# An attention and two gated feed-forward layers on one core: q's column norms taken over all partitions at once, before the softmax

## The chip, the cores and the metric

The kernel runs on one core of one Trainium2 chip. The metric is the device time of one execution in microseconds (us), smaller is better. Times of the kernel before are the median of three runs; the profile is of one more execution.

## The reference

Only the first stage matters here. q, k and v are 6016 x 256 in float32.

```
qn = q / (norm of each column of q + 1e-06)
kn = k / (norm of each column of k + 1e-06)
s  = kn.T @ qn / tau                  # 256 x 256
s  = s - s.max(-1);  a = exp(s);  a /= a.sum(-1) + 1e-09
x  = v @ a                            # 6016 x 256
x  = x / rms(x) * gain;  y = (silu(x @ w_gate) * (x @ w_val)) @ w_out      # layer 1, d_ff 1536
out = (sigmoid(y @ w2_gate) * (y @ w2_val)) @ w2_out                       # layer 2
```

## The kernel before, in words

Five instruction streams are written out by hand, each in its own order, and are tied by semaphores. TensorE (PE) does the products; float32 products run in two passes, and where it pays a matrix is split in a rounded high part and a low rest (float32r). VectorE (DVE) and ScalarE (ACT) do the elementwise work, GpSimd (POOL) a little, SyncE (SP) issues nearly all DMAs.

**The stream of q and k.** Twenty-four pieces of q and k come in. ACT squares them (L461), DVE adds the squares (L694, folded at L707), and PE adds each piece into the raw scores k.T @ q, which lie in two PSUM banks, RAW: 128 rows (c = 0) and 128 rows (c = 1) of 256 columns. The last four pieces (LATE) are done for c = 0 first; ahead of the last of them PE makes the column sums of the squares (`column_norms`, L1087): four small float32 products, each with 128 columns of squares as the held matrix and one column of ones moving, which leave 128x1 in each of four banks (L1093). When c = 0 is whole (`raw_done` 1), PE does c = 1 of the first late piece, waits for `soft_step` 2, spreads q's inverse norms over all partitions (`spread_columns`, L1078, two products with the identity), and does c = 1 of the three other pieces (`raw_done` 2).

**From the sums to the scale.** ACT takes the root of the 128x4 sums (L473); DVE refines it and inverts it: reciprocal (L808), product with the sums (L811), sum (L814), reciprocal (L817, `half_inv`), k's own scale (L820, `k_scale`). Each step waits for the one before it.

**The softmax, two row halves.** `score(0)` (L834) multiplies the spread norms in PSUM by an SBUF copy of the raw scores (made by ACT, L475), by k's scale, and keeps each row's maximum; L838 negates it. ACT takes the exponents (L526), DVE inverts the row sum (L844, L847), ACT writes the first half of a (L532). ACT also copies the spread norms to SBUF (L543) for `score(1)`, which reads the raw scores from PSUM. v's first block arrives in `v_in` and is turned by DVE in two halves, `turn_v(0, 0)` and `turn_v(0, 1)` (L667), each of which bumps `v_turned`; ACT rounds the second half (L443), DVE makes its low part (L685). PE's `first_x` (L1017) multiplies the first half of v by the first half of a in float32 (L1023), once `v_turned` is 1 and a's half is there, and then waits for the second half of a (L852, L857) for the products of L1028. The order on DVE is: k_scale, turn_v(0,0), score(0), turn_v(0,1), inverse_sum(0), score(1), vt_low(0,1), inverse_sum(1), second_a.

**Behind it.** `first_up` (L1042) is the first tile of layer 1; the row norms of block 0 come from `add_squares(0)` on DVE (L729) and `sum_squares` on PE (L1071). DVE's `turn_v(1, 0)` stands just ahead of `add_squares(0)`. On SP, `load_v(1)` (L317) waits for `v_turned` 2, and the remaining weight loads stand behind it. From there on the twelve blocks of 512 tokens go through both layers in an order that is the same before and after.

Of the kernel before, what the change touches and what calls it, by code (L numbers as in the profile page):

```python
# [26 lines left out]
ALU = mybir.AluOpType  # L27
ACT = mybir.ActivationFunctionType
AX_X = mybir.AxisListType.X

P = 128
# [10 lines left out]
LATE = (21, 22, 23, 20)  # L42
# [7 lines left out]
def build(nc, q, k, v, tau, rms_g, w1_gate, w1_val, w1_out, w2_gate, w2_val, w2_out, out):  # L50
    _, N, C = q.shape
    F = w1_gate.shape[1]
    CC = C // P
# [42 lines left out]
    def alternate(cols, h):  # L96

        return cols[:, h:C:CC]
# [5 lines left out]
    with ExitStack() as ctx:  # L104
# [3 lines left out]
        def sem(name):  # L108
            return ctx.enter_context(nc.semaphore(name))
# [11 lines left out]
        with ExitStack() as early:  # L121
            qk = early.enter_context(nc.sbuf_tensor("qk", [P, QK_SLOTS, 2, QK_TILES * C], F32))
            sq_qk = early.enter_context(nc.sbuf_tensor("sq_qk", [P, SQ_BUFS, 2, QK_TILES * C], F32))
            sum_sq = early.enter_context(nc.sbuf_tensor("sum_sq", [P, 2, QK_TILES * C], F32))
# [6 lines left out]
        ones = sb("ones", [P, P])  # L131
# [7 lines left out]
        scratch = sb("scratch", [P, CC, BLOCK])  # L139
        y1 = sb("y1", [P, CC, BLOCK])  # L140
# [9 lines left out]
        small = sb("small", [P, 64])  # L150
# [3 lines left out]
        ps = ctx.enter_context(nc.psum_tensor("ps", [P, 8, BLOCK], F32))  # L154
        GATE, VALUE = (0, 2), (1, 3)
        Y, X = (4, 5), (6, 7)
        RAW, NORM, SPREAD = (0, 1), (2, 3, 4, 5), 2
        sum_ps = ps[:, X[0]:X[1] + 1, :]
        square_sums = ps[:, NORM[0]:NORM[3] + 1, 0:1]

        gain = [cols_t[:, c * SQ:c * SQ + 1] for c in range(CC)]
        tau_c = cols_t[:, 2 * SQ:2 * SQ + 1]
        qk_hi = [w_hi["o1"][:, n * JG:(n + 1) * JG, :].rearrange("p (a t) c -> p a (t c)", a=2) for n in range(HI_BUFS)]

        seed = small[:, 0:4]
        seed_inv = small[:, 4:8]
        other = small[:, 40:44]
        twice_norm_e = small[:, 44:48]
        four_inv_tau = small[:, 52:53]
        unread = small[:, 48:49]  # L170
        tiny = halves[:, 0, 0:1]
        half_inv = small[:, 12:16]
        inv_tau = small[:, 16:17]
        k_scale = small[:, 18:20]
        neg_max = small[:, 22:24]
# [4 lines left out]
        ms = small[:, 32:36]  # L180
        rinv = small[:, 36:40]

        q_scale = y1[:, 0, 0:C]
        first_raw = y1[:, 0, C:2 * C]
        scores = y1[:, 1, :].rearrange("p (c m) -> p c m", c=CC)
        probs = h[:, 0, :].rearrange("p (c m) -> p c m", c=CC)
        first_a = scores[:, 0, :]
        sq = scratch
        mean, root_y, root_t, root_turned = (roots[0:SQ, i, :] for i in range(4))
        ROOT_STEPS = 9 + 3 * ROOT_ROUNDS  # L190
        late_root = y1[:, 1, :]
# [14 lines left out]
        raw_done, sums_folded = sem("raw_done"), sem("sums_folded")  # L206
        norms_made, root_seeded, root_refined = sem("norms_made"), sem("root_seeded"), sem("root_refined")
        first_hi_done = {w: sem(f"first_hi_{w}") for w in W[:2]}
        first_lo_done = {w: sem(f"first_lo_{w}") for w in W[:2]}
        soft_step, q_spread, q_scaled = sem("soft_step"), sem("q_spread"), sem("q_scaled")  # L210
        raw_copied = sem("raw_copied")
        scores_neg_max, exp_done, row_inv_ready = sem("scores_neg_max"), sem("exp_done"), sem("row_inv_ready")
        first_a_done, a_hi_done, a_lo_done = sem("first_a_done"), sem("a_hi_done"), sem("a_lo_done")
        first_a_hi_done, first_a_lo_done = sem("first_a_hi_done"), sem("first_a_lo_done")
# [207 lines left out]
        def _(act):  # L422
# [47 lines left out]
              .then_inc(first_hi_done["g1"], 1)  # L470
            act.wait_ge(const_ready, 4)
            act.wait_ge(norms_made, 1)
            nc.scalar.activation(seed.unsqueeze(2), square_sums, ACT.Sqrt, bias=tiny).then_inc(root_seeded, 1)  # L473
            act.wait_ge(raw_done, 1)
            nc.scalar.activation(first_raw, ps[:, RAW[0], 0:C], ACT.Copy).then_inc(raw_copied, 1)  # L475
            act.wait_ge(table_loaded, 1)
            nc.scalar.activation(unread, ones[:, 0:1], ACT.Exp).then_inc(table_loaded, 1)

# [59 lines left out]
                  .then_inc(a_hi_done, 1)  # L538

            exponents(0)  # L540
            act.wait_ge(q_spread, 1)
            act.wait_ge(soft_step, 4)
            nc.scalar.activation(q_scale, ps[:, SPREAD, 0:C], ACT.Copy).then_inc(q_scaled, 1)  # L543
            first_a_scaled()
            vt_high(0, 1, x2)
            exponents(1)
# [102 lines left out]
        def _(dve):  # L649
# [13 lines left out]
            def turn_v(b, c):  # L663
                w = width(b)
                if c == 0:
                    dve.wait_ge(v_loaded, b * 16 * QUARTERS + 16 * QUARTERS)
                nc.vector.transpose(x_raw[:, c, 0:w].rearrange("p (s t) -> p s t", t=SQ),  # L667
                                    v_in[:, 0:w // SQ, c:C // QUARTERS:CC]).then_inc(v_turned, 1)
# [131 lines left out]
            def x2_low(b, c, dst):  # L800
# [7 lines left out]
            nc.vector.reciprocal(seed_inv, seed).then_inc(root_refined, 1)  # L808
            dve.wait_ge(root_refined, 1)
            dve.wait_ge(norms_made, 1)  # L810
            nc.vector.tensor_tensor(other.unsqueeze(2), square_sums, seed_inv.unsqueeze(2), ALU.mult)\  # L811
              .then_inc(root_refined, 1)
            dve.wait_ge(root_refined, 2)
            nc.vector.scalar_tensor_tensor(out=twice_norm_e, in0=other, scalar=2e-6, in1=seed, op0=ALU.add, op1=ALU.add)\  # L814
              .then_inc(soft_step, 1)
# [1 line left out]
            nc.vector.reciprocal(half_inv, twice_norm_e).then_inc(soft_step, 1)  # L817
            dve.wait_ge(soft_step, 2)
            dve.wait_ge(cols_made, 4)
            nc.vector.tensor_scalar(k_scale, half_inv[:, 2:4], four_inv_tau, None, ALU.mult).then_inc(soft_step, 1)  # L820
            turn_v(0, 0)
            dve.wait_ge(soft_step, 3)

            def score(c):

                if c:
                    dve.wait_ge(q_scaled, 1)
                    dve.wait_ge(raw_done, 2)
                    in_psum, in_sbuf = ps[:, RAW[1], 0:C], q_scale
                else:  # L830
                    dve.wait_ge(raw_copied, 1)
                    dve.wait_ge(q_spread, 1)
                    in_psum, in_sbuf = ps[:, SPREAD, 0:C], first_raw
                nc.vector.tensor_tensor_reduce(out=scores[:, c, :], in0=in_psum, in1=in_sbuf,  # L834
                                               scale=k_scale[:, c:c + 1], scalar=LOWEST, op0=ALU.mult, op1=ALU.max,
                                               accum_out=row_max[:, c:c + 1]).then_inc(soft_step, 1)
                dve.wait_ge(soft_step, 2 * c + 4)
                nc.vector.tensor_scalar(neg_max[:, c:c + 1], row_max[:, c:c + 1], -1.0, None, ALU.mult)\  # L838
                  .then_inc(scores_neg_max, 1)

            def inverse_sum(c):

                dve.wait_ge(exp_done, c + 1)
                nc.vector.tensor_scalar(row_sum_e[:, c:c + 1], row_sum[:, c:c + 1], 1e-9, None, ALU.add)\  # L844
                  .then_inc(soft_step, 1)
                dve.wait_ge(soft_step, 2 * c + 5)
                nc.vector.reciprocal(row_inv[:, c:c + 1], row_sum_e[:, c:c + 1]).then_inc(row_inv_ready, 1)  # L847
# [11 lines left out]
                                                   op0=ALU.mult, op1=ALU.subtract).then_inc(a_lo_done, 1)  # L859

            score(0)
            turn_v(0, 1)
            inverse_sum(0)
            score(1)
            vt_low(0, 1, x2)
            inverse_sum(1)
# [5 lines left out]
            for back in range(2):  # L872
                for d in range(CC):
# [3 lines left out]
                                                   in1=xs[0][:, d, tokens].bitcast(F32), op0=ALU.mult, op1=ALU.subtract)\  # L877
# [115 lines left out]
        def _(pe):  # L993
# [81 lines left out]
            def spread_columns(bank, cols, n):  # L1075

                for i in range(n):
                    mm = nc.tensor.matmul(ps[:, bank, i * P:(i + 1) * P], cols[:, i:i + 1].broadcast_to([P, P]),  # L1078
                                          ident[:, :], start=True, stop=True)
                return mm  # L1080
# [6 lines left out]
            def column_norms():  # L1087

                pe.wait_ge(sums_folded, 1)
                for part in range(2):  # L1090
                    cols = sum_sq[:, part, 0:C]
                    for c in range(CC):
                        mm = nc.tensor.matmul(ps[:, NORM[2 * part + c], 0:1],  # L1093
                                              alternate(cols, c) if part else cols[:, c * P:(c + 1) * P],
                                              ones[:, 0:1], start=True, stop=True)
                mm.then_inc(norms_made, 1)

            def warm_up(n):

# [4 lines left out]
            def raw(i, c, first=0, end=QK_TILES):  # L1104

                _, slot, t0, n = chunks[i]
                dst = ps[:, RAW[c], 0:C]
                for t in range(first, min(end, n)):
                    cols = slice(t * C, (t + 1) * C)
                    if i in SPLIT:  # L1110
                        buf = qk_hi[SPLIT.index(i) % HI_BUFS]
                        q_hi, q_lo = buf[:, 0, cols], qk_lo[:, slot, 0, cols]
                        k_hi, k_lo = buf[:, 1, cols], qk_lo[:, slot, 1, cols]
                        nc.tensor.matmul(dst, alternate(k_hi, c), q_hi, start=False, stop=False)  # L1114
                        nc.tensor.matmul(dst, alternate(k_hi, c), q_lo, start=False, stop=False)  # L1115
                        mm = nc.tensor.matmul(dst, alternate(k_lo, c), q_hi, start=False,  # L1116
                                              stop=(i == LATE[-1] and t == n - 1))
                    else:
                        mm = nc.tensor.matmul(dst, alternate(qk[:, slot, 1, cols], c), qk[:, slot, 0, cols],  # L1119
                                              start=(t0 + t == 0), stop=(i == LATE[-1] and t == n - 1))  # L1120
                return mm
# [14 lines left out]
            for n, i in enumerate(LATE):  # L1136
# [2 lines left out]
                parts_ready(i)  # L1139
                mm = raw(i, 0)  # L1140
            mm.then_inc(raw_done, 1)
            raw(LATE[0], 1)
            pe.wait_ge(soft_step, 2)
            spread_columns(SPREAD, half_inv, CC).then_inc(q_spread, 1)
            for i in LATE[1:]:
                mm = raw(i, 1)
            mm.then_inc(raw_done, 1)
            first_x()
# [144 lines left out]
```

## Time and profile before

| what | value |
|---|---|
| median of 3 runs | 1240.8 us (1240.49 to 1240.97) |
| the profiled execution's own time | 1240.53 us |
| its span (first to last instruction) | 1238.6 us |
| PE busy in the span | 1231.8 us (99%) |
| mean granted TensorE clock | 0.999 |

The span leaves 1.9 us of the profiled execution outside. In the profile a line number is that of the kernel above; a float32 product counts as two matmul instructions, one for each pass. The times in the timeline are from the span's start, with the duration behind them.

### The profile page before, as it was taken

To read this page: it belongs to the slowest core of one execution; us is meant where nothing else is said; L and a number is where in the kernel's file an instruction comes from. 1 tells how busy PE (TensorE), PEld (TensorE's weight loads), DVE (VectorE), ACT (ScalarE), POOL (GpSimd) and SP (SyncE) were. 2 spreads that over 40 slices of the span, in tenths; PEclk is the share of its full clock that TensorE was granted. 3 is DMA by queue.
4 is the path that set the end of the run, shared out by engine and by line. 5 is a ranking of instruction groups with operands and counts; after the bars stand their busy time and mean duration, and the time that the engine had idled before them with its cause. 6 is when DMAs were issued, how large, how long until landed. Compare 5 with 4: busy or idle time off the path is not lost.

```text
span 1238.6 us, 15730 instructions
## 1 busy us (share of the span) xinstructions
PE 1231.8 (99%) x5614; PEld 1036.9 (84%) x5614; DVE 684.6 (55%) x1152; ACT 463.2 (37%) x765; POOL 57.5 (5%) x40
## 2 busy tenths in 40 slices
PE   9999999999999999999999999999999999999998
PEld 8888888888888888888888888888888888889888
DVE  7896655554554555555555455455555555545333
ACT  7755433333333333333333333333333333333332
POOL 7203400000000000000000000000000000000000
PEclk9999999999999999999999999999999999999999
DMA  9930000000100100100000010010010000000000
GB/s 357 302 93 14 1 9 18 18 0 9 34 0 9 34 0 9 34 0 9 17 17 0 9 34 0 9 34 0 9 34 0 9 17 13 1 7 18 1 18 13
DMA packets 65478, 37.28 MB, mean 30 GB/s; under 512 B 51756, under 2 KB 55212, under 8 KB 65452
## 3 DMA queue, kind: packets, MB, share of 16 engines
q1 hardware_dynamic: 64344, 36.34, 10.3%
q10 hardware_dynamic: 1108, 0.59, 0.2%
q8 instruction: 16, 0.26, 0.1%
q14 instruction: 10, 0.08, 0.0%
HBM read 30.74 MB, written 6.18 MB: 30 GB/s over the span
## 4 chain that ended last, share of the span: by engine, by line
PE 99%; DMA 0%; SPq 0%; DVE 0%; issue 0%; ACT 0%; DVEq 0%
PE ps L1002 21%; PE ps L1004 21%; PE ps L1003 21%; PE ps L1192 10%; PE ps L1190 10%; PE ps L1191 10%; PE ps L1119 2%; DMA qk<-in_k 0%; PE ps L1114 0%; PE ps L1116 0%; PE ps L1115 0%; SPq L299 0%; PE ps L1028 0%; PE ps L1071 0%; PE ps L1078 0%; DVE out_sb L679 0%
## 5 line engine op out<-in xcount | busy, mean ns | idle before, releaser
L935 DVE TENSOR_TENSOR h<-ps,h 128x512 f32<-128x512 f32 (+1 forms) x276 | 187.7, 680 | 249.2 <-PE ps L1004 236.6
L597 ACT ACTIVATE h_hi<-h 128x512 fp32r<-128x512 f32 (+1 forms) x276 | 171.5, 621 | 362.8 <-DVE h L935 362.8
L592 ACT ACTIVATE h<-ps 128x512 f32<-128x512 f32 (+1 forms) x276 | 162.2, 588 | 329.5 <-PE ps L1004 317.9
L940 DVE TENSOR_TENSOR h_lo<-h,h_hi 128x512 fp32r<-128x512 f32 (+1 forms) x276 | 187.8, 681 | 139.0 <-ACT h_hi L597 137.2
L1192 PE MATMUL ps<-h_hi,w_lo_o 128*128 128x512 f32 (+1 forms) x576 | 221.6, 385 | 0.0
L1190 PE MATMUL ps<-h_hi,w_hi_o 128*128 128x512 f32 (+1 forms) x576 | 221.5, 385 | 0.0
L1191 PE MATMUL ps<-h_lo,w_hi_o 128*128 128x512 f32 (+1 forms) x576 | 221.5, 385 | 0.0
L931 DVE TENSOR_TENSOR h<-ps,h 128x512 f32<-128x512 f32 (+1 forms) x132 | 89.7, 679 | 138.5 <-ACT h L592 138.5
L1192 PEld LDWEIGHTS ps<-h_hi,w_lo_o 128*128 128x128 f32 x576 | 108.1, 188 | 20.6
L1190 PEld LDWEIGHTS ps<-h_hi,w_hi_o 128*128 128x128 f32 x576 | 108.1, 188 | 20.6
L1191 PEld LDWEIGHTS ps<-h_lo,w_hi_o 128*128 128x128 f32 x576 | 108.1, 188 | 20.6
L1002 PE MATMUL ps<-xs_hi,w_hi_g 128*128 128x512 f32 (+1 forms) x310 | 118.2, 381 | 0.0
L1002 PE MATMUL ps<-xs_hi,w_hi_v 128*128 128x512 f32 (+1 forms) x310 | 118.1, 381 | 0.0
L1004 PE MATMUL ps<-xs_hi,w_lo_g 128*128 128x512 f32 (+1 forms) x310 | 118.0, 381 | 0.0
L1003 PE MATMUL ps<-xs_lo,w_hi_g 128*128 128x512 f32 (+1 forms) x310 | 118.0, 381 | 0.0
L1004 PE MATMUL ps<-xs_hi,w_lo_v 128*128 128x512 f32 (+1 forms) x310 | 118.0, 381 | 0.0
L1003 PE MATMUL ps<-xs_lo,w_hi_v 128*128 128x512 f32 (+1 forms) x310 | 118.0, 380 | 0.0
L1004 PE MATMUL ps<-x_hi,w_lo_g 128*128 128x512 f32 x264 | 102.8, 389 | 0.0
L1003 PE MATMUL ps<-x_lo,w_hi_g 128*128 128x512 f32 x264 | 102.7, 389 | 0.0
L1003 PE MATMUL ps<-x_lo,w_hi_v 128*128 128x512 f32 x264 | 102.7, 389 | 0.0
L1004 PE MATMUL ps<-x_hi,w_lo_v 128*128 128x512 f32 x264 | 102.7, 389 | 0.0
L1002 PE MATMUL ps<-x_hi,w_hi_v 128*128 128x512 f32 x264 | 102.7, 389 | 0.0
(170 smaller groups left out, 1396.8 us busy)
## 6 DMA issues: line engine op xcount, KB each, us to landing
qk<-in_q SPq DMA_DIRECT2D x23, 256.0 KB, 7.4
qk<-in_k SPq DMA_DIRECT2D x22, 256.0 KB, 8.2
v_in<-in_v SPq DMA_DIRECT2D x44, 128.0 KB, 3.0
out<-out_sb SPq DMA_DIRECT2D x44, 128.0 KB, 2.4
w_raw_g<-in_moe_w_gate SPq DMA_DIRECT2D x6, 512.0 KB, 9.2
w_raw_v<-in_moe_w_val SPq DMA_DIRECT2D x6, 512.0 KB, 9.8
w_raw_o<-in_moe_w_out SPq DMA_DIRECT2D x6, 512.0 KB, 9.2
scratch<-root_row SPq DMA_DIRECT2D x10, 256.0 KB, 3.1
```

The source lines that it names most:

```text
L592: nc.scalar.activation(h[:, slot, 0:w], ps[:, GATE[slot], 0:w], ACT.Sigmoid).then_inc(sig_done, 1)
L597: nc.scalar.activation(h_hi[:, part, 0:w], h[:, slot, 0:w], ACT.Copy).then_inc(hi_done, 1)
L931: nc.vector.tensor_tensor(h[:, slot, 0:w], ps[:, GATE[slot], 0:w], h[:, slot, 0:w], ALU.mult).then_inc(gated_done, 1)
L935: nc.vector.tensor_tensor(h[:, slot, 0:w], ps[:, VALUE[slot], 0:w], h[:, slot, 0:w], ALU.mult).then_inc(h_done, 1)
L940: nc.vector.tensor_tensor(h_lo[:, part, 0:w], h[:, slot, 0:w], h_hi[:, part, 0:w].bitcast(F32), ALU.subtract).then_inc(lo_done, 1)
L1002: nc.tensor.matmul(dst, s_hi, m_hi, start=(n == 0), stop=False)
L1003: nc.tensor.matmul(dst, s_hi, m_lo, start=False, stop=False)
L1004: mm = nc.tensor.matmul(dst, s_lo, m_hi, start=False, stop=(n == last))
L1119: mm = nc.tensor.matmul(dst, alternate(qk[:, slot, 1, cols], c), qk[:, slot, 0, cols], start=(t0 + t == 0), stop=(i == LATE[-1] and t == n ...
L1190: nc.tensor.matmul(dst, hi, h_hi[:, part, 0:w], start=(j == 0), stop=False)
L1191: nc.tensor.matmul(dst, hi, h_lo[:, part, 0:w], start=False, stop=False)
L1192: return nc.tensor.matmul(dst, lo, h_hi[:, part, 0:w], start=False, stop=(j == J - 1))
```

## The change

q's sums of squares are no longer made as a column and spread later. PE multiplies a held 128x128 matrix of ones by the 256 columns of squares, so that every partition holds all of q's 256 sums; k's two columns of sums stand beside them in the same bank, 258 columns in all. Root, reciprocal, refinement and second reciprocal then run over 128x258 instead of 128x4. The result is q's scale on all partitions, in SBUF, so that PE's spread with its wait, ACT's copy of the raw scores and ACT's copy of the spread norms are gone. Both halves of v's first block are turned behind `score(0)`, one ahead of the first row sum's inverse and one behind it.

```
-        RAW, NORM, SPREAD = (0, 1), (2, 3, 4, 5), 2
-        square_sums = ps[:, NORM[0]:NORM[3] + 1, 0:1]
+        RAW, NORM = (0, 1), 2
+        square_sums = ps[:, NORM, 0:C + CC]
...
-        half_inv = small[:, 12:16]
-        first_raw = y1[:, 0, C:2 * C]
+        half_inv = y1[:, 0, 0:C + CC]
+        q_scale = half_inv[:, 0:C]
+        seed, seed_inv = scratch[:, 0, 0:C + CC], scratch[:, 1, 0:C + CC]
+        other, twice_norm_e = seed_inv, seed
...
-            nc.scalar.activation(seed.unsqueeze(2), square_sums, ACT.Sqrt, bias=tiny).then_inc(root_seeded, 1)
-            act.wait_ge(raw_done, 1)
-            nc.scalar.activation(first_raw, ps[:, RAW[0], 0:C], ACT.Copy).then_inc(raw_copied, 1)
+            nc.scalar.activation(seed, square_sums, ACT.Sqrt, bias=tiny).then_inc(root_seeded, 1)
...
-            act.wait_ge(q_spread, 1)
-            act.wait_ge(soft_step, 4)
-            nc.scalar.activation(q_scale, ps[:, SPREAD, 0:C], ACT.Copy).then_inc(q_scaled, 1)
...
-            nc.vector.tensor_tensor(other.unsqueeze(2), square_sums, seed_inv.unsqueeze(2), ALU.mult)\
-              .then_inc(root_refined, 1)
+            nc.vector.tensor_tensor(other, square_sums, seed_inv, ALU.mult).then_inc(root_refined, 1)
...
-            nc.vector.tensor_scalar(k_scale, half_inv[:, 2:4], four_inv_tau, None, ALU.mult).then_inc(soft_step, 1)
-            turn_v(0, 0)
+            nc.vector.tensor_scalar(k_scale, half_inv[:, C:C + CC], four_inv_tau, None, ALU.mult).then_inc(soft_step, 1)
...
-                nc.vector.tensor_tensor_reduce(out=scores[:, c, :], in0=in_psum, in1=in_sbuf,
+                dve.wait_ge(raw_done, c + 1)
+                nc.vector.tensor_tensor_reduce(out=scores[:, c, :], in0=ps[:, RAW[c], 0:C], in1=q_scale,
...
             score(0)
+            turn_v(0, 0)
+            inverse_sum(0)
             turn_v(0, 1)
-            inverse_sum(0)
             score(1)
...
-                for part in range(2):
-                    cols = sum_sq[:, part, 0:C]
-                    for c in range(CC):
-                        mm = nc.tensor.matmul(ps[:, NORM[2 * part + c], 0:1],
-                                              alternate(cols, c) if part else cols[:, c * P:(c + 1) * P],
-                                              ones[:, 0:1], start=True, stop=True)
+                for c in range(CC):
+                    nc.tensor.matmul(ps[:, NORM, C + c:C + c + 1], alternate(sum_sq[:, 1, 0:C], c), ones[:, 0:1],
+                                     start=True, stop=True)
+                nc.tensor.matmul(ps[:, NORM, 0:C], ones[:, :], sum_sq[:, 0, 0:C], start=True, stop=True)\
+                  .then_inc(norms_made, 1)
...
-            raw(LATE[0], 1)
-            pe.wait_ge(soft_step, 2)
-            spread_columns(SPREAD, half_inv, CC).then_inc(q_spread, 1)
-            for i in LATE[1:]:
+            for i in LATE:
                 mm = raw(i, 1)
```

## Rows read from the trace of the kernel before

**Rows 1.** The page: busy time, share of the span and instructions of each engine

```profile
PE 1231.8 (99%) x5614; PEld 1036.9 (84%) x5614; DVE 684.6 (55%) x1152; ACT 463.2 (37%) x765; POOL 57.5 (5%) x40
```

**Rows 2.** Chain that ended last, 36 to 56 us: start us, us, what

```profile
39.52 0.81 PE ps L1093 x8
...
42.02 0.45 PE ps L1078 x4
42.47 1.73 PE ps L1119 x8
...
44.80 0.13 PE ps L1116
...
47.24 1.67 PE ps L1028 x12
```

**Rows 3.** Timeline, 30 to 54 us: start us, us, engine, line, instruction, idle before

```profile
40.42 0.26 ACT L473 ACTIVATE small<-ps,halves 128x4 f32<-128x4 f32 x1 [1.71 <-PE ps L1093]
40.72 0.18 DVE L808 RECIPROCAL small<-small 128x4 f32<-128x4 f32 x1 [0.39 <-ACT small L473]
...
41.54 0.23 DVE L820 TENSOR_SCALAR small<-small 128x2 f32<-128x2 f32 x1
...
42.66 0.48 DVE L834 CUSTOM_DVE_ANT_0 y<-ps,y,small 128x256 f32<-128x256 f32 x1
...
43.25 0.70 DVE L667 STREAM_TRANSPOSE x_raw<-v_in 128x512 f32<-128x512 f32 x1
...
44.39 0.51 ACT L532 ACTIVATE y<-h,small 128x256 f32<-128x256 f32 x1
...
44.81 0.61 ACT L443 ACTIVATE x_hi<-x_raw 128x512 fp32r<-128x512 f32 x1
...
45.05 1.97 PE L1023 MATMUL ps<-x_raw,y 128*128 128x256 f32 x8
45.07 0.48 DVE L834 CUSTOM_DVE_ANT_0 y<-ps,y,small 128x256 f32<-128x256 f32 x1 [0.71 <-PE ps L1116]
...
45.66 0.68 DVE L685 TENSOR_TENSOR x_lo<-x_raw,x_hi 128x512 fp32r<-128x512 f32 x1
...
46.42 0.15 DVE L844 TENSOR_SCALAR small<-small 128x1 f32<-128x1 f32 x1
```

**Rows 4.** Groups by shape, DVE, 0 to 60 us: busy us, mean ns, idle before

```profile
L870 DVE TENSOR_TENSOR a_lo<-y,a_hi 128x256 fp32r<-128x256 f32 x1 | 0.4, 417 | 0.0
L847 DVE RECIPROCAL small<-small 128x1 f32<-128x1 f32 x2 | 0.3, 164 | 0.1
...
L844 DVE TENSOR_SCALAR small<-small 128x1 f32<-128x1 f32 x2 | 0.3, 154 | 0.1
...
L808 DVE RECIPROCAL small<-small 128x4 f32<-128x4 f32 x1 | 0.2, 178 | 0.4 <-ACT small L473 0.4
...
L814 DVE SCALAR_TENSOR_TENSOR small<-small 128x4 f32<-128x4 f32 x1 | 0.2, 161 | 0.0
```

**Rows 5.** Groups by shape, ACT, 0 to 60 us

```profile
L496 ACT ACTIVATE xs_hi<-ps,cols_t 128x256 fp32r<-128x256 f32 x4 | 1.6, 477 | 0.3 <-PE ps L1028 0.3
...
L473 ACT ACTIVATE small<-ps,halves 128x4 f32<-128x4 f32 x1 | 0.3, 263 | 1.7 <-PE ps L1093 1.7
```

**Rows 6.** v's second block: its DMAs (timeline, tile v_in), first reader on DVE

```profile
43.98 2.58 SPq L317 DMA_DIRECT2D v_in<-in_v  x4
...
L317 SPq DMA_DIRECT2D v_in<-in_v x8: 572/682/3242, 28.8 to 45.9; - x8
...
DMA to landing us min/median/max: 2.7/4.9/10.2
...
50.19 0.70 DVE L667 STREAM_TRANSPOSE x_raw<-v_in 128x512 f32<-128x512 f32 x1
```

**Rows 7.** Timeline, PE's weight loads: the product behind the squares' sum

```profile
51.62 0.52 PEld L1071 LDWEIGHTS ps<-ones,scratch 128*128 128x128 f32 x4 [0.25 <-DVE scratch L729]
```

**Rows 8.** Stretches: us, busy of PE, PEld, DVE, ACT, POOL, clock, DMA share, GB/s

```profile
9.00:10.00 1.00, 0.53 (x2) 0.51 (x3) 0.90 (x2) 0.71 (x2) 0.84 (x2) 1.00 1.08 410
```

More of the change, by code:

```diff
@@ L163, in build @@
         qk_hi = [w_hi["o1"][:, n * JG:(n + 1) * JG, :].rearrange("p (a t) c -> p a (t c)", a=2) for n in range(HI_BUFS)]
[L165 to L168, printed above, removed]
         four_inv_tau = small[:, 52:53]
@@ L181, in build @@
         rinv = small[:, 36:40]
-        q_scale = y1[:, 0, 0:C]
-        first_raw = y1[:, 0, C:2 * C]
+        half_inv = y1[:, 0, 0:C + CC]
+        q_scale = half_inv[:, 0:C]
         scores = y1[:, 1, :].rearrange("p (c m) -> p c m", c=CC)
@@ L209, in build @@
         first_lo_done = {w: sem(f"first_lo_{w}") for w in W[:2]}
-        soft_step, q_spread, q_scaled = sem("soft_step"), sem("q_spread"), sem("q_scaled")
-        raw_copied = sem("raw_copied")
+        soft_step = sem("soft_step")
         scores_neg_max, exp_done, row_inv_ready = sem("scores_neg_max"), sem("exp_done"), sem("row_inv_ready")
@@ L819, in _ @@
             dve.wait_ge(cols_made, 4)
-            nc.vector.tensor_scalar(k_scale, half_inv[:, 2:4], four_inv_tau, None, ALU.mult).then_inc(soft_step, 1)
-            turn_v(0, 0)
+            nc.vector.tensor_scalar(k_scale, half_inv[:, C:C + CC], four_inv_tau, None, ALU.mult).then_inc(soft_step, 1)
             dve.wait_ge(soft_step, 3)
             def score(c):
[L826 to L833, printed above, removed]
-                nc.vector.tensor_tensor_reduce(out=scores[:, c, :], in0=in_psum, in1=in_sbuf,
+                dve.wait_ge(raw_done, c + 1)
+                nc.vector.tensor_tensor_reduce(out=scores[:, c, :], in0=ps[:, RAW[c], 0:C], in1=q_scale,
                                                scale=k_scale[:, c:c + 1], scalar=LOWEST, op0=ALU.mult, op1=ALU.max,
@@ L1089, in column_norms @@
                 pe.wait_ge(sums_folded, 1)
-                for part in range(2):
-                    cols = sum_sq[:, part, 0:C]
-                    for c in range(CC):
-                        mm = nc.tensor.matmul(ps[:, NORM[2 * part + c], 0:1],
-                                              alternate(cols, c) if part else cols[:, c * P:(c + 1) * P],
-                                              ones[:, 0:1], start=True, stop=True)
-                mm.then_inc(norms_made, 1)
+                for c in range(CC):
[3 more added lines that the diff above has]
+                  .then_inc(norms_made, 1)
             def warm_up(n):
```

## The prediction

> **What bounds the kernel now.** I read the page first: PE is busy 99% of the span [rows 1], so a change outside PE counts only by how long it makes PE stand still, or by the PE work it takes away. Next came the chain that ended last, cut to the stretch of the change. The reader is to see that it stays on PE through the norms, the spread and the raw scores of c = 1, whose last pass ends at 44.80 + 0.13 = 44.93 us, then leaves PE for the second half of the softmax, and is back on PE at 47.24 with the products of L1028 [rows 2]. Then the timeline of all engines from 30 to 54 us. It shows what runs beside that: PE does first_x's float32 products from 45.05 to 47.02, so it stands still only about 0.1 us before them and 0.2 us behind them. score(1) starts at 45.07 after 0.71 us idle on DVE, because c = 1 of the raw scores came last [rows 3]. Here the softmax and PE are nearly balanced: a longer chain on ACT or DVE is paid almost in full, and a shorter one gains at most some 0.3 us. Everything behind 47.24 is the same work in the same order, so the start of L1028 is my measure: its shift is the change of the time, unless something behind it comes late by more.
>
> **Part by part, PE.** The norms took 0.81 us for eight passes [rows 2], 0.10 each. k's four stay (0.40). q's four become two passes over 256 columns; L1119 does eight such in 1.73 us [rows 2], 0.216 each, so 0.43. The sum is 0.83: +0.02. The spread's 0.45 us goes; its wait for soft_step cost nothing. So raw_done 2 comes at 44.93 - 0.45 + 0.02 = 44.50.
>
> **The root.** ACT's root of 128x4 took 0.263; over 258 columns the nearest row is L496, 256 columns from PSUM with a pointer operand, 0.477 [rows 5]: +0.21. ACT's two copies (L475, L543) go. Neither ended a wait that counts, so I take nothing for them. The exponent's table load moves ahead of where it stood and stays hidden.
>
> **The two ordinary DVE steps.** Product and sum went at 161 ns over 4 columns; over 256, L870 takes 417 [rows 4]. That is +0.26 each, +0.52 together.
>
> **The two reciprocals** are the open price: no row has a wide one. One column took 164 ns, four took 178 [rows 4], 14 ns for three columns, 4.7 ns a column. Ordinary steps grow by (417 - 161)/252 = 1.02 ns a column. Carried on, R = 178 + 254 x 4.7 = 1.36 us. The bounds: at the ordinary rate R is 178 + 254 x 1.02 = 0.44 us, and I can't exclude that the 14 ns are a fixed cost of a short instruction, since 154 ns for one column and 161 for four in ordinary ones differ by 7 too [rows 4]. From above, three columns that partly hide in the fixed part could cost up to eight ordinary columns each, 8.1 ns: R = 2.24 us. I take 1.36, the only growth measured on this instruction. The reciprocals then add 2 x (1.36 - 0.178) = 2.36 us.
>
> VectorE: DVE Perf Modes, a page of the Trainium skill (section "Walkthrough: the 8-slice pipeline in each mode"), says that the reciprocal is an iterative divide with a repeat count of 8. Read as eight cycles a column it speaks for the upper bound and against this change, and by it the sum below would be 4.09 us instead of 2.33; the 14 ns of the trace are only about half of it. No row here settles it.
>
> **The chain on DVE.** Before, k_scale ended at 41.54 + 0.23 = 41.77, and score(0) began at 42.66, behind a turn of v and the spread [rows 3]. After, k_scale ends at 41.77 + 0.02 + 0.21 + 0.52 + 2.36 = 44.88 and score(0) follows at 44.91: +2.25. The 0.89 us of slack that the turn filled are used up in this. Behind score(0) the first turn takes the slot that the second had (43.25, 0.70, until the exponents are done), so the first half of a and with it first_x's start keep their distance: 45.05 + 2.25 = 47.30. The second turn now stands behind the inverse: DVE is free for it when ACT's L532 starts, 44.39 - 42.66 = 1.73 us behind score(0)'s start, and it takes 0.70 [rows 3]. So score(1) starts at 44.91 + 1.73 + 0.70 = 47.34, give or take the issue gaps: +2.27. It no longer waits for PE.
>
> Queued behind that later turn: ACT's rounding of the turned half (0.61) can start only at 47.36, ends at 47.97, and DVE's low part, which stood 0.59 behind score(1)'s start (45.66 against 45.07), now stands some 0.7 behind it. It takes 0.68, and the row sum's inverse stood 1.35 behind score(1)'s start (46.42) [rows 3]: at about 0.7 + 0.68 = 1.4 it is late by 0.06. Start of L1028: +2.27 + 0.06 = **+2.33 us**, at 49.57. first_x's products are over by then (47.30 + 1.97 = 49.27).
>
> **Behind it.** SP's load of v's second block waits for the second turn: it was issued from 43.98, now from 47.37, +3.39, while its reader moves by 2.33 only. The last of the four DMAs was issued at 45.9 and its reader ran unheld at 50.19, so it landed within 4.3 us; the quickest took 2.7 [rows 6]. After, it lands between 52.0 and 53.6, and the reader wants it at 52.52. That is 0 to 1.1 us late. What it would hold is add_squares(0), for which PE already waited 0.25 us [rows 7]. I take the short landing, since nothing else is queued ahead of it on SP, cost it at nothing, and keep up to 1.1 us for the range. The weight loads behind it on SP move by 3.4 us too. No wait for a weight shows up behind 50 us, and I cost them at nothing.
>
> **The sum**: +0.02 +0.21 +0.52 +2.36 in the chain, less 0.89 of slack, is +2.22; issue gaps, the moved turn and the late low part add 0.11: +2.33. Against the profiled execution's 1240.53 that is 1242.86. The median of the runs is 0.27 higher, so I say 1243.1. With the reciprocal open: change = 2.33 + 2 x (R - 1.36).
>
> **The rivals.**
>
> (a) *The reciprocal is as cheap per column as an ordinary step*, R = 0.44. For it: ordinary instructions of 1 to 4 columns differ by 7 ns as well, so a slope from such short ones is weak. Against it: both reciprocals of four columns read 178, and the form is the same. The change is then +0.49, 1241.3 us: no change. It decides this side for R below 1.43.
>
> (b) *The reciprocal repeats its step eight times a column*, R = 2.24. For it: the short forms may hide part of the growth. Against it: three more columns would be 24 ns, and 14 are seen. The change is +4.09, 1244.9 us, slower. The page named above is the rule for it.
>
> (c) *The clock falls.* PE now stands still from 44.50 to 47.30, 2.8 us, where before it had 0.1. In the trace the granted clock stays at 1.00 (2.4 GHz) through the thinnest stretch, 0.53 us of work in 1 us [rows 8], but there is no gap as long as this. If the clock goes to 1.2 GHz for first_x alone, its 1.73 us become 3.5 and L1028 starts 1.2 us later still: +3.5, 1244.3 us. If L1028's 1.67 go at half clock as well it is +5.2, 1246.0. With R = 2.24 the gap is 4.6 us and this is likelier.
>
> (d) *v's second block comes late*: +0.5 to +1.1 on top of the forecast, 1243.6 to 1244.2 us.
>
> A gain needs less than nothing: with reciprocals as short as before, the formula gives -0.03 us. I leave 2 in 100 for it.
>
> **How the numbers follow.** About 0.2% (2.5 us) is what a measurement of this kernel tells from no change. Forecast (R from 1.1 to 1.7, clock held, v in time) 0.50; (a) 0.16; (b) 0.14, with or without the clock; (c) alone 0.08; (d) 0.10; faster 0.02. The forecast, +2.33, lies just inside 0.2%: R above 1.43 puts it outside, and its own range, 1242.6 to 1243.8, straddles the bound, so I split it 0.25 and 0.25. Slower: 0.25 + 0.14 + 0.08 + 0.08 of (d) = 0.55. Same: 0.25 + 0.16 + 0.02 = 0.43. The range takes in (a), (d), (b) and the first form of (c): 1241.1 to 1245.3.
>
> **What would show it.** In the changed profile: L1093's successors end near 40.35; the root takes 0.47; the two wide reciprocals read 1.36 us each (0.44 under (a), 2.24 under (b)); score(0) at 44.9, score(1) at 47.3 with DVE not waiting for PE; PE idle for 2.8 us ahead of L1023 and some 0.3 behind it; L1028 at 49.6; L667 of the second block without a wait; granted clock 1.00 from 44 to 52. The prediction is wrong if the reciprocal has another rate, if the clock drops in the gap, or if first_x's products rather than the second half of a turn out to be what L1028 waits for.

## The result and the profile after

The changed kernel takes 1245.21 us (median of 8 runs, 1244.09 to 1245.98) against 1240.81 (1240.49 to 1241.86): 4.40 us more, ratio 1.0035, 95% interval 1.0025 to 1.0044. It is slower, beyond the 0.2% that a measurement tells from no change. The forecast was 1243.1, with a range of 1241.1 to 1245.3. The direction held. The range held by 0.1 us, and three of the eight runs lie above it; nearly half of the loss was not in the forecast's sum. The profiled execution took 1245.66 us with a span of 1243.7, the kernel before 1240.53 with 1238.6: 5.1 us apart.

The line numbers are now those of the changed kernel. Its timeline from 38.5 to 58 us answers to [rows 3]:

```profile
40.62 0.48 ACT L469 ACTIVATE scratch<-ps,halves 128x258 f32<-128x258 f32 x1 [1.92 <-PE ps L1076]
...
41.13 1.77 DVE L799 RECIPROCAL scratch<-scratch 128x258 f32<-128x258 f32 x1 [0.78 <-ACT scratch L469]
...
42.93 0.43 DVE L802 TENSOR_TENSOR scratch<-ps,scratch 128x258 f32<-128x258 f32 x1
43.39 0.43 DVE L804 SCALAR_TENSOR_TENSOR scratch<-scratch 128x258 f32<-128x258 f32 x1
...
43.85 1.77 DVE L807 RECIPROCAL y<-scratch 128x258 f32<-128x258 f32 x1
...
45.66 0.23 DVE L810 TENSOR_SCALAR small<-y,small 128x2 f32<-128x2 f32 x1
45.92 0.48 DVE L816 CUSTOM_DVE_ANT_0 y<-ps,y,small 128x256 f32<-128x256 f32 x1
...
48.15 0.44 DVE L816 CUSTOM_DVE_ANT_0 y<-ps,y,small 128x256 f32<-128x256 f32 x1
...
48.30 3.75 PE L1006 MATMUL ps<-x_raw,y 128*128 128x256 f32 x8 [3.77 <-DVE x_raw L658]
...
49.91 0.29 DVE L834 TENSOR_SCALAR a_hi<-h,small 128x128 fp32r<-128x128 f32 x1
```

Two things are to be seen. The two reciprocals take 1.77 us each. And first_x's eight passes, the same work as in [rows 3], take 3.75 us instead of 1.97, after PE stood still for 3.77. (The profile names the second turn of v, L658, as what released them. By the kernel they wait for the first turn and for the first half of a, and ACT ended that half at 47.65 + 0.51 = 48.16.) The chain that ended last, in the same stretch, answers to [rows 2]:

```profile
39.62 0.36 PE ps L1074 x4
39.98 0.55 PE ps L1076 x2
...
45.92 0.48 DVE y L816
...
48.30 3.75 PE ps L1006 x8
52.06 2.04 PE ps L1011 x12
54.09 0.12 PE ps L1034
```

The norms start 0.10 us later than before (39.62 against 39.52), which is the spread of the stream of q and k. The second half of a is ready at 49.91 + 0.29 = 50.20, and with the 0.14 us that stood between it and PE before, L1011 could start at 50.34, 3.10 later than L1028 before. But it waits for first_x's slow passes until 52.06, and takes 2.04 us instead of 1.67. The next product starts at 54.09; before, L1028 ended at 47.24 + 1.67 = 48.91: +5.18 us, which is the whole difference of the spans. So 3.1 us are the longer chain, and 2.1 are what happened to PE. The stretches show what that was; the sixth number (behind the five engines) is the granted clock:

```profile
45.50:46.00 0.50, 0.00 (x0) 0.00 (x0) 0.43 (x3) 0.00 (x0) 0.00 (x0) 1.00 0.00 0
46.00:46.50 0.50, 0.00 (x0) 0.00 (x0) 0.47 (x3) 0.00 (x0) 0.00 (x0) 0.98 0.00 0
46.50:47.00 0.50, 0.00 (x0) 0.00 (x0) 0.50 (x2) 0.37 (x1) 0.00 (x0) 0.50 0.00 0
...
52.50:53.00 0.50, 0.50 (x4) 0.50 (x4) 0.00 (x0) 0.00 (x0) 0.00 (x0) 0.50 0.80 97
53.00:53.50 0.50, 0.50 (x5) 0.50 (x5) 0.00 (x0) 0.34 (x1) 0.00 (x0) 0.69 0.68 106
53.50:54.00 0.50, 0.50 (x7) 0.50 (x6) 0.33 (x1) 0.50 (x2) 0.00 (x0) 1.00 0.77 299
```

PE had no work from 44.54 on. The clock was 1.00 (2.4 GHz) until some 2 us into that, then 0.50 (1.2 GHz) until about 53.3, through all of first_x and most of L1011. In the runs this differs: the fastest of the eight, 1244.09, had a mean clock of 1.000 and lies 3.3 us above the median of before, about what the longer chain alone would give; the profiled one had 0.996. Only the profiled execution shows the clock stretch by stretch. For the others there is the mean over the whole run. There 0.999 and 1.000 tell little, since the kernel before has both; 0.998 and less it never has, and four of the eight runs here do.

### The profile page after: what moved, and what is told of

Its sections match the earlier page's. It is cut to its first block, busy times and chain, and to the rows that moved or that the text cites. A ratio compares the mean times of both kernels' runs of the same rounds, so it can differ in the third digit from the quotient of the medians.

```text
span 1243.7 us, 15714 instructions
## 1 busy us (share of the span) xinstructions
PE 1233.7 (99%) x5608; PEld 1038.5 (84%) x5608; DVE 688.2 (55%) x1152; ACT 462.8 (37%) x763; POOL 57.6 (5%) x40
## 4 chain that ended last, share of the span: by engine, by line
PE 98%; DVE 1%; DMA 0%; SPq 0%; ACT 0%; issue 0%; ACTq 0%
PE ps L985 21%; PE ps L986 21%; PE ps L987 21%; PE ps L1168 10%; PE ps L1170 10%; PE ps L1169 10%; PE ps L1100 1%; DMA qk<-in_k 0%; PE ps L1095 0%; PE ps L1096 0%; PE ps L1097 0%; PE ps L1006 0%; SPq L295 0%; PE ps L1011 0%; DVE y L807 0%; DVE scratch L799 0%
```

## The experiments

The kernels ran beside the kernel before; its median was 1240.92 us for the first four, 1241.02 for the next four and 1241.12 for the last two.

**PE kept busy in the gap** (e1).

```
                 mm = raw(i, 1)
             mm.then_inc(raw_done, 1)
+            warm_up(14)
             first_x()
```

> The changed kernel, with 14 more float32 products of 128x128 constants on PE between the last raw scores and first_x. They fill about 3.1 of the 3.7 us in which PE stood still, and nothing reads them. Theory (the two wide reciprocals cost 3.1 us, and the clock that falls in the gap costs the rest): the granted clock stays at 1.00 from 44 to 54 us, L1011's successor starts 3.1 us later than in the kernel before, and the time is 1243.9 us, 1.3 under the changed kernel's 1245.2, with less spread from run to run. Rival (the rest comes from v's second block or the weight loads, moved back on SP's queue): the time stays at 1245.2 whatever the clock does.

Measured: 1244.10 us (9 runs, 1243.71 to 1244.89), ratio 1.0025 [1.0015, 1.0035]. That is 1.1 under the changed kernel's median, as the theory had it within 0.2. Its stretches and its chain:

```profile
46.00:47.00 1.00, 1.00 (x11) 1.00 (x10) 0.93 (x5) 0.06 (x1) 0.00 (x0) 1.00 0.00 0
...
49.00:50.00 1.00, 1.00 (x7) 0.87 (x6) 0.86 (x3) 1.00 (x4) 0.00 (x0) 1.00 0.02 6
```

```profile
39.93 0.36 PE ps L1074 x4
...
48.61 1.97 PE ps L1006 x8
...
50.66 1.66 PE ps L1011 x12
```

With the clock at 1.00, first_x takes 1.97 us again, and L1011 starts 50.66 - 47.24 = 3.42 us later than before, 0.41 of it because the norms already started 0.41 later (39.93 against 39.52): 3.0 for the chain. Adding 3.3 us of unread work to PE made the kernel faster. The rival, a late v or late weights, fell: nothing of SP's order was touched.

**Only the order of v's turns** (e2), on the kernel before.

```
-            turn_v(0, 0)
             dve.wait_ge(soft_step, 3)
...
             score(0)
+            turn_v(0, 0)
+            inverse_sum(0)
             turn_v(0, 1)
-            inverse_sum(0)
```

> The kernel before, with only the order of v's turns changed: both behind score(0), as in the changed kernel. Theory: score(0) starts at 42.5 instead of 42.66 us, the second turn ends near 44.9, score(1) still starts near 45.1 because the raw scores of c = 1 come last, and the time is 1240.8, within 0.3. Rival (the second turn on the path costs its 0.7 us and moves the load of v's second block by 1 us): 1241.5 or more.

Measured: 1240.89 us (11 runs), ratio 0.9999 [0.9990, 1.0008]. As the theory had it: the order of the turns costs nothing there. The load of v's second block was issued at 45.24 us instead of 43.98, and its first reader waited 0.21 us for it in the profile; the time doesn't show it.

**One wide reciprocal** (e3). The inverse of the root is refined by itself.

```
-                    nc.vector.tensor_scalar(four_inv_tau, inv_tau, 4.0, None, ALU.mult).then_inc(cols_made, 1)
+                    nc.vector.tensor_scalar(four_inv_tau, inv_tau, 1.0, None, ALU.mult).then_inc(cols_made, 1)
...
-            nc.vector.tensor_tensor(other, square_sums, seed_inv, ALU.mult).then_inc(root_refined, 1)
+            nc.vector.tensor_tensor(twice_norm_e, square_sums, seed_inv, ALU.mult).then_inc(root_refined, 1)
             dve.wait_ge(root_refined, 2)
-            nc.vector.scalar_tensor_tensor(out=twice_norm_e, in0=other, scalar=2e-6, in1=seed, op0=ALU.add, op1=ALU.add)\
-              .then_inc(soft_step, 1)
+            nc.vector.scalar_tensor_tensor(out=twice_norm_e, in0=twice_norm_e, scalar=-0.5, in1=seed_inv, op0=ALU.mult,
+                                           op1=ALU.mult).then_inc(soft_step, 1)
             dve.wait_ge(soft_step, 1)
-            nc.vector.reciprocal(half_inv, twice_norm_e).then_inc(soft_step, 1)
+            nc.vector.scalar_tensor_tensor(out=half_inv, in0=twice_norm_e, scalar=1.5, in1=seed_inv, op0=ALU.add,
+                                           op1=ALU.mult).then_inc(soft_step, 1)
```

> The changed kernel with one wide reciprocal instead of two: the root's inverse is refined by a Newton step (one product, two scalar-tensor-tensor steps), and the second reciprocal goes; the 1e-06 beside the norms is left out. In the chain 1.77 us go and one more step of 0.44 comes in place of it: 1.33 us less, PE idle for 2.4 us instead of 3.7. Theory (reciprocals by width, clock by the gap): 1242.6 us if the clock holds in the shorter gap, 1243.6 to 1244 if it still falls. Rival (the softmax's two wide ordinary steps, or the moved turns, carry the loss): the time stays above 1244.5.

Measured: 1243.88 us (11 runs), ratio 1.0019 [1.0010, 1.0029]. The runs fall in two groups: three at 1242.2 to 1242.6, eight at 1243.7 to 1244.4. The profiled one, 1244.42, is of the second; its timeline and its stretches:

```profile
47.85 2.76 PE L1007 MATMUL ps<-x_raw,y 128*128 128x256 f32 x8 [2.43 <-DVE x_raw L658]
```

```profile
47.00:48.00 1.00, 0.15 (x1) 0.18 (x2) 1.00 (x3) 0.70 (x2) 0.00 (x0) 1.00 0.00 0
48.00:49.00 1.00, 1.00 (x5) 0.90 (x6) 0.84 (x4) 1.00 (x4) 0.00 (x0) 0.94 0.00 0
49.00:50.00 1.00, 1.00 (x4) 0.72 (x4) 0.90 (x5) 0.83 (x3) 0.00 (x0) 0.50 0.64 146
```

PE was idle for 2.4 us up to 47.85; the clock fell only a microsecond after it had gone back to work. Here it cost 1.3 us: L1012 could have started at 49.89 and started at 50.61, and took 2.22 us instead of 1.67. (The norms started 0.7 us later than in the kernel before as well, at 40.23.) So the same kernel has both outcomes that I had named, and the lower group lies 1.5 us below the upper one. That the clock makes the groups is a reading: one profile shows it, and of the other seven upper runs three have a mean clock of 0.998 and four 0.999.

**Reciprocals by width** (e4). Ten of them, and five products with a constant, in a row on DVE before anything else. They were put into the changed kernel, not into the kernel before as the expectation says; all of them run before the first sum, so nothing of the change is under way yet.

```
+            widths, tried = (1, 2, 4, 8, 16, 32, 64, 128, 258, 512), sem("widths")
+            nc.vector.memset(y1[:, :, :], 3.0).then_inc(tried, 1)
+            for n, cols in enumerate(widths):
+                dve.wait_ge(tried, n + 1)
+                nc.vector.reciprocal(y1[:, 1, 0:cols], y1[:, 0, 0:cols]).then_inc(tried, 1)
...
```

> The kernel before, with ten reciprocals of 1, 2, 4, 8, 16, 32, 64, 128, 258 and 512 columns, and five products with a constant of 1, 4, 16, 64 and 258 columns, in a row on DVE ahead of its first sum. The time of the whole says nothing; the durations do. Theory (6.3 ns a column from a few columns on, whatever the operands): 16 columns 0.25 us, 64 columns 0.55, 128 columns 0.96, 258 columns 1.77, 512 columns 3.36, while the short ones, 1 to 4, stay near 0.16 to 0.18. Rival (the 1.77 us come from the place of the operands or from other engines' traffic in the changed kernel): 258 columns take 1.4 us or less here.

Its time (1252.5 us) says nothing; the groups by shape on DVE from 0 to 12.3 us do (busy us, mean ns):

```profile
L683 DVE RECIPROCAL y<-y 128x512 f32<-128x512 f32 x1 | 3.4, 3354 | 0.0
L683 DVE RECIPROCAL y<-y 128x258 f32<-128x258 f32 x1 | 1.8, 1766 | 0.0
...
L683 DVE RECIPROCAL y<-y 128x128 f32<-128x128 f32 x1 | 1.0, 953 | 0.0
...
L683 DVE RECIPROCAL y<-y 128x16 f32<-128x16 f32 x1 | 0.3, 253 | 0.0
L683 DVE RECIPROCAL y<-y 128x8 f32<-128x8 f32 x1 | 0.2, 203 | 0.0
...
L683 DVE RECIPROCAL y<-y 128x4 f32<-128x4 f32 x1 | 0.2, 178 | 0.0
...
L683 DVE RECIPROCAL y<-y 128x2 f32<-128x2 f32 x1 | 0.2, 166 | 0.0
L683 DVE RECIPROCAL y<-y 128x1 f32<-128x1 f32 x1 | 0.2, 164 | 0.0
```

From 8 columns on each column costs 6.25 ns: (253 - 203)/8 and (3354 - 1766)/254 alike. From 2 to 4 it costs 6 each, from 1 to 2 only 2. So the nine from 2 to 512 columns lie within 1 ns of one line, 153 + 6.25 ns a column, and the single column lies 5 ns above it (164 against 159). The width alone makes the 1.77 us; its place and its neighbours have no part in it, and the rival (1.4 us or less) is out. Of the products with a constant, 258 columns took 295 ns and 16 took 174; the one of 4 took 974 ns, against 154 for one column, and no run says why.

**v's first turn in the wait for the root** (e5), on the changed kernel.

```
+            turn_v(0, 0)
             dve.wait_ge(root_seeded, 1)
...
             score(0)
-            turn_v(0, 0)
+            turn_v(0, 1)
             inverse_sum(0)
-            turn_v(0, 1)
             score(1)
```

> The changed kernel, with v's first turn moved from behind score(0) to where DVE waits for ACT's root (0.78 us idle in the changed kernel's profile), and the second turn ahead of the first row sum's inverse, as in the kernel before. Theory (the turns are no part of the loss, because first_x waits for the first half of a and its float32 products then take as long as the second half of the softmax): score(0) stays at 45.9 us, first_x at 48.3, and the time stays at 1245.2, within 0.3. Rival (the 0.7 us that the second turn stands ahead of score(1) is paid in full): 1244.5.

Measured: 1247.13 us (4 runs, 1246.55 to 1247.87), ratio 1.0048 [1.0033, 1.0064]. Both theories missed. The timeline:

```profile
41.72 0.48 ACT L469 ACTIVATE scratch<-ps,halves 128x258 f32<-128x258 f32 x1 [2.56 <-PE ps L1076]
42.81 0.71 DVE L658 STREAM_TRANSPOSE x_raw<-v_in 128x512 f32<-128x512 f32 x1 [1.70 <-DMA v_in<-in_v]
43.44 1.72 DVE L800 RECIPROCAL scratch<-scratch 128x258 f32<-128x258 f32 x1
```

The root was done at 42.20 in this execution, and DVE could not take it, because the turn ahead of it waited for v's first block, which landed at 42.8. From 42.22 to 43.44 that is 1.2 us on the path. I had looked at when DVE is free and not at when the data is there. The rest of this execution is the stream of q and k: ACT's root started at 41.72 against 40.62 in the changed kernel's profile, 1.1 us later, and 1.2 + 1.1 is what first_x is late by (50.58 against 48.30). The clock fell here too, at about 48.6, 3.0 us into PE's gap. The median of the four runs is 1.9 us over the changed kernel's; whether the stream was late in all four, and whether the edit has a part in that, isn't shown.

**Both, with PE kept busy** (e7): the edits of e3 and e5, and

```
             mm.then_inc(raw_done, 1)
+            warm_up(9)
             first_x()
```

> The best form of the changed kernel that these reasons give: one wide reciprocal with a Newton step in place of two (the 1e-06 beside the norms left out), v's first turn in the wait for the root, and 9 unread float32 products of 128x128 on PE in the gap ahead of first_x. Theory (a wide reciprocal at 1.77 us stays in the chain, and the clock is held): the granted clock stays at 1.00, first_x starts near 46.9, and the time is 1242.2 to 1242.6, with no run at 1243.7 or more, so still 1.5 us over the kernel before. Rival (the clock fell for another reason than the gap): the times stay in two groups as with one reciprocal alone.

Measured: 1243.28 us (11 runs, 1242.81 to 1244.44), ratio 1.0019 [1.0010, 1.0028]. That is 0.7 over the upper end of what was expected, and two runs (1243.95 and 1244.44) lie where none should. The clock held in the profile; v's block was on the chain that ended last again:

```profile
36.06 5.90 DMA v_in<-in_v
```

It landed at 41.96. ACT's root was done at 41.80 and the reciprocal, behind the turn, began at 42.62: 0.8 us lost. So I took the early turn out.

**One wide reciprocal, PE kept busy** (e10): the edit of e3 and the `warm_up(9)` of e7; v's turns as in the changed kernel.

> One wide reciprocal with the Newton step (the 1e-06 beside the norms left out) and 9 unread float32 products of 128x128 on PE in the gap ahead of first_x; v's turns stay where the changed kernel has them. Theory (the two groups of times seen with one reciprocal alone are the clock held and the clock fallen; the version with the early turn lost 0.7 us to the late landing of v's first block): one group at 1242.2 to 1242.8, clock 1.00 in the gap. Rival (something else than the clock makes two groups): two groups again, at 1242.4 and 1243.9.

Measured: 1242.75 us (11 runs, 1242.23 to 1243.84), ratio 1.0014 [1.0005, 1.0023]. Eight of eleven lie within 1242.2 and 1243.0, and the group at 1243.7 to 1244.4 has shrunk from eight runs to two. These two weren't expected, and one of them, 1243.84, is the profiled one. Its clock is 1.00; the profile shows something else. Its chain:

```profile
40.80 0.36 PE ps L1075 x4
...
54.96 1.05 PE ps L1055 x8
```

The norms start 1.28 us later than in the kernel before (39.52), because the stream of q and k up to them ran later. L1012 starts at 50.18, which is 2.94 later than L1028 did: 1.28 of the stream and 1.66 of the chain with one wide reciprocal. Then comes something smaller:

```profile
53.62 0.71 DVE L658 STREAM_TRANSPOSE x_raw<-v_in 128x512 f32<-128x512 f32 x1 [0.40 <-DMA v_in<-in_v]
```

```profile
54.95 0.97 PEld L1055 LDWEIGHTS ps<-ones,scratch 128*128 128x128 f32 x8 [0.64 <-DVE scratch L720]
```

That is rival (d): v's second block is late by 0.40 us, and PE waits 0.64 for the squares' sum instead of 0.25 [rows 7]. L1055 starts 3.15 us later than L1071 before (51.81), so (d) adds 0.2 to the 2.94. In the changed kernel the same reader had no wait, in e1 neither. The late stream is thus the larger part of what sets this run apart. The other one, 1243.73, has a mean clock of 1.000 as well; what delayed it isn't shown. A time of 1243.7 or more doesn't by itself say that the clock fell.

**Short reciprocals** (e8), on the changed kernel.

```
+            preset = sem("preset")
+            nc.vector.memset(seed_inv, 1.0).then_inc(preset, 1)
+            nc.vector.memset(half_inv, 1.0).then_inc(preset, 1)
...
-            nc.vector.reciprocal(seed_inv, seed).then_inc(root_refined, 1)
+            dve.wait_ge(preset, 2)
+            nc.vector.reciprocal(seed_inv[:, C - 2:C + 2], seed[:, C - 2:C + 2]).then_inc(root_refined, 1)
...
-            nc.vector.reciprocal(half_inv, twice_norm_e).then_inc(soft_step, 1)
+            nc.vector.reciprocal(half_inv[:, C - 2:C + 2], twice_norm_e[:, C - 2:C + 2]).then_inc(soft_step, 1)
```

> The changed kernel with both reciprocals over 4 of the 258 columns (the last two of q's and k's two); the other 254 keep ones that are written beforehand, so q's norms are left out but for two columns. All else is as in the changed kernel: norms by ones, root, product and sum over 258 columns, no spread, no copies, v's turns behind score(0). Theory (what costs is the width of the reciprocals and the clock in the gap that they make): the reciprocals take 0.18 us each, score(0) starts near 42.8, PE hardly stands still, the clock holds, and the time is 1240.8, within 0.3, as the sum of the prediction gives it for free reciprocals. Rival (the wide root, product and sum cost what they take, 0.7 us): 1241.5 or more.

Measured: 1241.30 us (11 runs, 1240.59 to 1241.70), ratio 1.0001 [0.9992, 1.0010]. Its chain:

```profile
40.19 0.40 PE ps L1078 x4
...
48.07 1.66 PE ps L1015 x12
```

L1015 starts 0.83 us later than L1028 did, of which 0.67 were there already at the norms (40.19 against 39.52). Everything in the change but the width of the reciprocals costs 0.2 to 0.3 us; the interval holds zero. The time lies between the two expectations: 0.2 above the theory's 1241.1 and 0.2 below the rival's 1241.5. Against the kernel before that ran beside it (1241.02) it is the theory's, and the clock held.

**Half of the gap filled** (e9), on the changed kernel.

```
             mm.then_inc(raw_done, 1)
+            warm_up(7)
             first_x()
```

> The changed kernel with 7 unread float32 products of 128x128 right behind the last raw scores, 1.6 us of work, so that PE stands still for some 2.2 us ahead of first_x instead of 3.7. Theory (the clock falls by how long PE stands still): it falls in fewer runs than in the changed kernel, and where it holds the time is 1243.7 to 1244.3; where it falls 1245 or more. If the times are all at 1244, a gap of 2.2 us is short enough; if they are all near 1245.2, it isn't.

Measured: 1244.50 us (7 runs), ratio 1.0031 [1.0020, 1.0043]. Five runs at 1243.9 to 1244.7, two at 1245.4 and 1246.1, and one of those two has a mean clock of 0.998, the lowest of the seven. Only the profiled run, 1243.87, shows the clock stretch by stretch, and there it held. PE stood still for 2.21 us there. It fits the theory, with few runs to carry it: two of the five are above the 1244.3 that it allowed, and a late stream of q and k (e10) could make the two slow ones as well.

**The delay alone** (e11), on the kernel before: two unread reciprocals behind the first narrow one.

```
+            unread_done = sem("unread_done")
+            nc.vector.memset(scratch[:, :, 0:C + CC], 3.0).then_inc(unread_done, 1)
...
             nc.vector.reciprocal(seed_inv, seed).then_inc(root_refined, 1)
+            for n in range(2):
+                dve.wait_ge(unread_done, n + 1)
+                nc.vector.reciprocal(scratch[:, 1, 0:C + CC], scratch[:, 0, 0:C + CC]).then_inc(unread_done, 1)
```

> The kernel before, with nothing of the change, and two unread reciprocals of 258 columns on DVE behind the first narrow one. They push soft_step 2 back by 3.6 us, and PE, which waits for it behind the first late piece, stands still for 3.2 us. Theory (a gap of some 3 us on PE is enough for the clock to fall, whatever makes it): the granted clock goes to 0.5 about 2 us into the gap or soon after it, PE's spread and late pieces run at half speed behind it, and the time is 1246 to 1247. Rival (the clock falls for a reason of the changed kernel's own): the clock holds at 1.00, and the time is 1240.9 + 3.6 = 1244.5.

Measured: 1246.03 us (5 runs), ratio 1.0036 [1.0022, 1.0050]; four at 1245.4 to 1246.6, one at 1243.69 with a mean clock of 1.000. The profile is of a run at 1245.44:

```profile
45.06 0.71 PE L1083 MATMUL ps<-ident,small 128*128 128x128 f32 x4 [2.82 <-DVE small L822]
```

```profile
45.50:46.00 0.50, 0.50 (x5) 0.48 (x4) 0.42 (x2) 0.00 (x0) 0.00 (x0) 1.00 0.00 0
46.00:47.00 1.00, 1.00 (x4) 0.85 (x4) 0.96 (x4) 0.33 (x1) 0.00 (x0) 0.66 0.00 0
47.00:48.00 1.00, 1.00 (x5) 0.76 (x3) 0.57 (x3) 0.85 (x4) 0.00 (x0) 0.50 0.00 0
```

PE stood still for 2.82 us, went back to work, and about 1.3 us later the clock fell, as the theory had it. It needs nothing of the change. The one run at 1243.69 came out 0.8 under the 1244.5 that I had written for a clock that holds. The profile gives the likely reason: the time grows by how long PE stands still, 2.82 us, and not by the 3.6 us of the two reciprocals, since PE had work of its own (L1124) until 42.24, behind which the first part of the delay is hidden; 1241.12 + 2.82 = 1243.9, against 1243.69.

## Why the prediction was right or wrong

The direction and the path were right, and that the time came to lie inside the range was in part luck. The reciprocals cost 0.8 us more than was taken and the fallen clock 1.1 us more in the medians (2.1 in the profile). The two together came to 0.1 us from the range's edge, and no rival priced this pair: (b) has a still longer reciprocal, (c) the fallen clock alone.

**What bounds the kernel**: right. A longer chain in this stretch was paid in full: 3.1 us at L1011 and again in the span where the clock held.

**The norms**: 0.36 + 0.55 = 0.91 us instead of 0.83; q's two passes over 256 columns took 0.55 instead of 0.43, k's four 0.36 instead of 0.40. **The root**: 0.48, as taken (0.477). **The two ordinary steps**: 427 and 429 ns, taken as 417. **The spread gone, raw_done 2 at 44.5**: right, PE's last raw score ends at 44.54.

**The reciprocals**: the first step that failed. "Carried on, R = 178 + 254 x 4.7 = 1.36 us" measured 1.77. The 4.7 ns were the slope between one column and four. e4 shows that only the single column lies off the line: 2 ns for the second column, 6 each for the third and fourth, and 6.25 from there on. The upper bound had allowed for such a thing. The mis-sized term is worth 2 x 0.41 = 0.82 us, and with it the forecast's own formula gives 2.33 + 0.82 = 3.15; the chains of the changed kernel and of e1, less what their norms came late, show 3.0. What is less than 3.15 is the way from score(0) to score(1), 48.15 - 45.92 = 2.23 us where 2.43 was taken, set against norms that took 0.08 more. The mechanism and the rest of the sum stand. The Trainium skill's repeat count of 8 (VectorE: DVE Perf Modes, "Walkthrough: the 8-slice pipeline in each mode") had pointed the right way, to a cost far over an ordinary step's; read as eight cycles a column it is too much. By the 0.96 GHz that the same page of the Trainium skill gives for VectorE (section "The TRN2 errata — SBUF-src ops pay a fixed extra latency per instruction"), the measured 6.25 ns would be six cycles, an estimate.

**"Clock held"**: the second step that failed, and the larger one where it did. It was rival (c) with 0.08. I had found the gap (2.8 us by the sum, 3.77 in the profile) and priced the fall rightly in kind: where the forecast had L1028 start 1.2 us later for a slow first_x, L1011 started 1.7 later than it could have (52.06 against 50.34), and was itself 0.4 longer. It is also the sign that the prediction had named, that first_x's products and not the second half of a are what L1028's successor waits for. What I got wrong was its chance. I took the clock's hold through a stretch with 0.53 us of work in 1 us [rows 8] as support, and that row has no gap of 2 us in it. e1 shows it from one side, e11 from the other. The two steps are not independent: 0.82 of the 0.97 us by which the gap came out longer are the dearer reciprocals.

**Rival (a)** is out: 0.44 against 1.77 us. **Rival (b)** gave 1244.9, next to the measured 1245.21, but for the wrong reason: R is 1.77, not 2.24, and the clock makes up the difference. **Rival (d)** did not occur in the changed kernel, where the fallen clock moved the reader back by 2 us more; in e1, where the clock held, it did not occur either: the last part was issued at 50.5 and its reader started unheld at 53.61. It shows in e10, with a wait of 0.40 us, inside its price of 0 to 1.1, of which 0.2 reach the time.

**The turns**: right. e2 shows that moving them costs nothing in the kernel before, and e5 why at least one of them is better off behind the score: v's first block landed only at 42.8 us in that execution.

No version tried here beats the kernel before; the best with the wide norms, e10, is 1.6 us over it. Whether the wide norms could gain anything with no wide reciprocal at all stays open; e8, which leaves that work out, says that there is nothing measurable to win.

## What to carry to other kernels

A slope taken from instructions of one to four columns was too low here (4.7 ns a column against 6.25), because the shortest one lay above the line of the others. So price a widened operation by a row of its own width, or measure it by itself, as e4 does, before the forecast. When a change makes TensorE wait longer at one place, ask what the clock does behind the gap: here gaps of 2.4 to 3.8 us cost 1 to 2 us more in part or most of the runs, and unread products in the gap bought it back. Before work is moved into an engine's idle time, look up when its data lands. And before two single executions are compared, look at where they stand ahead of the change: between the profiled ones here the norms started at anything from 39.5 to 40.8 us, and in e5 and e10 that went into the time in full.

## What was not expected of the hardware

The reciprocal on VectorE costs 6.25 ns a column, about six times the 1.02 ns of an ordinary step over two operands, but only 2 ns for the second one (164, 166, 178 ns for 1, 2, 4).

The clock can fall after the gap is over: in e3 it fell 1 us after PE had resumed and in e11 1.3 us after, in both cases behind gaps of under 3 us; in the changed kernel it fell 2 us into the gap, in e5 3 us into it. Whether it falls differs from run to run of one kernel (by their times three of eleven runs escaped in e3, one of five in e11), which also widens the spread of the times: 1.9 us from lowest to highest in the changed kernel, 1.2 with the gap filled.
